# Attention, gated convolution and MLP on one core: Q, K and V laid out by kernel(), keys read in place for the first batch

## The reference

```
# attention: block 32, window 16
k_sum = k.reshape(B, H, nb, 32, D).max(axis=3)
v_sum = v.reshape(B, H, nb, 32, D).mean(axis=3)
local   = scale * q @ k.T          where |i - j| < 16, else -1e9
summary = scale * q @ k_sum.T + log(32)
a = softmax([local, summary]);   x = a @ [v, v_sum]
# gated convolution, x is (2, 768, 512), d_ff 1024
h = relu(x @ w_in);  g = sigmoid(conv3(h, conv_w));  x = (h * g) @ w_out
# MLP, 4 * 512 = 2048 hidden
out = x + relu(layernorm(x) * g_ln @ w_ch1) @ w_ch2
```

## Time and profile before

| what | before |
|---|---|
| median of three runs | 463.69 us |
| span of the profiled execution | 460.9 us |
| instructions | 8619 |
| DMA in all | 35.28 MB in 74725 packets, of which 57632 under 512 B |
| PE busy | 452.0 us |

### The profile page before, as it was taken

The page is one execution under the profiler, slowest core; times in us unless marked ns, Lnnn a source line. Parts: engine busy times, 40 slices in busy tenths (PEclk is TensorE's granted clock), DMA queues, the critical chain, the costliest instruction groups (busy, mean ns, idle before and its releaser), DMA issues.

```text
span 460.9 us, 8619 instructions
## 1 busy us (share of the span) xinstructions
PE 452.0 (98%) x3114; PEld 400.5 (87%) x3114; DVE 275.0 (60%) x630; ACT 200.1 (43%) x503; POOL 268.3 (58%) x405
## 2 busy tenths in 40 slices
PE   7899999999999999999999999999999999999997
PEld 6687888989989889989889988998998899889885
DVE  4999976876666967974674254546762244124333
ACT  3898997433335746436243143422421233123210
POOL 2559689999945000097898889750042687878000
PEclk9999999999999999999999999999999999999999
DMA  9998951212102000002115324120020211220003
GB/s 229 213 232 197 195 140 53 92 47 91 47 0 93 0 1 0 1 0 91 54 41 143 109 93 93 67 91 1 26 89 23 93 46 47 91 93 0 1 0 137
DMA packets 74725, 35.28 MB, mean 77 GB/s; under 512 B 57632, under 2 KB 68924, under 8 KB 74684
## 3 DMA queue, kind: packets, MB, share of 16 engines
q1 hardware_dynamic: 71164, 33.85, 27.1%
q10 hardware_dynamic: 3520, 0.88, 0.9%
HBM read 28.83 MB, written 3.15 MB: 69 GB/s over the span
## 4 chain that ended last, share of the span: by engine, by line
PE 96%; DMA 1%; DVE 1%; issue 1%; ACT 1%; ACTq 0%; DVEq 0%
PE two L1689 10%; PE two L1687 10%; PE two L1688 10%; PE two L1664 9%; PE two L1667 8%; PE two L1666 8%; PE two L1460 5%; PE two L1462 5%; PE two L1461 5%; PE two L1595 5%; PE two L1596 5%; PE two L1594 5%; PE two L1413 3%; PE two L1445 3%; PE two L1424 3%; PE two L1342 3%
## 5 line engine op out<-in xcount | busy, mean ns | idle before, releaser
L640 POOL TENSOR_TENSOR asum<-wst 128x256 f32<-128x256 f32 x26 | 21.8, 838 | 93.4 <-PE two L1462 50.2
L1664 PE MATMUL two<-combo,wa 128*128 128x384 f32 x224 | 75.8, 338 | 0.0
L1667 PE MATMUL two<-combo,wa 128*128 128x384 f32 x224 | 75.6, 337 | 0.0
L1666 PE MATMUL two<-combo,wa 128*128 128x384 f32 x224 | 75.2, 336 | 0.0
L1689 PE MATMUL two<-wv,h 128*128 128x512 f32 x192 | 75.0, 391 | 0.0
L1687 PE MATMUL two<-wv,h 128*128 128x512 f32 x192 | 74.8, 390 | 0.2 <-DVE h L946 0.2
L1688 PE MATMUL two<-wv,h 128*128 128x512 f32 x192 | 75.0, 390 | 0.0
L1023 DVE TENSOR_TENSOR u<-two,u 128x384 f32<-128x384 f32 x16 | 8.9, 558 | 90.2 <-PE two L1667 90.2
L1267 ACT ACTIVATE h<-u 128x384 fp32r<-128x384 f32 x16 | 8.4, 525 | 122.4 <-DVE u L1023 122.4
L574 POOL TENSOR_SCALAR pn<-ex,rinv 128x120 f32<-128x120 f32 x96 | 34.8, 383 | 19.1 <-DVE rinv L736 18.4
L634 POOL TENSOR_TENSOR wa<-asum,wa 128x256 fp32r<-128x256 f32 x52 | 43.2, 831 | 4.3
(11 more groups left out here) (119 smaller groups left out, 981.0 us busy)
## 6 DMA issues: line engine op xcount, KB each, us to landing
wst<-in_moe_w_ch SPq DMA_DIRECT2D x26, 512.0 KB, 3.2
vW<-in_v SPq DMA_DIRECT2D x13, 288.0 KB
kn<-in_k SPq DMA_DIRECT2D x15, 192.0 KB, 3.8
qn<-in_q SPq DMA_DIRECT2D x15, 192.0 KB, 3.7
out<-y SPq DMA_DIRECT2D x11, 256.0 KB, 2.0
wst<-in_moe_w_in SPq DMA_DIRECT2D x8, 256.0 KB, 3.1
wst<-in_moe_w_out SPq DMA_DIRECT2D x8, 256.0 KB, 2.8
tok<-xq SPq DMA_DIRECT2D x32, 48.0 KB, 2.0
```

Source lines behind the costliest of these rows:

```text
L1664: nc.tensor.matmul(o, wk[:, 0, kk], ck[:, 0, kk], start=(first and kk == 0), stop=False, skip_group_check=True)
L1666: nc.tensor.matmul(o, wk[:, 0, kk], ck[:, 1, kk], start=False, stop=False, skip_group_check=True)
L1667: ins = nc.tensor.matmul(o, wk[:, 1, kk], ck[:, 0, kk], start=False, stop=(kk == 1), skip_group_check=True)
```

## The change

kernel() now hands over other arrays: Q and K with two heads' 64 dimensions on 128 rows and tokens along the row (K with 16 zeros at each end), V as the 96-row windows of its 12 blocks packed in one row per partition (6 KB), conv_w and g_ln with 128 rows. So `keys_t`, `queries_t`, `queries`, `window_keys_0`, the transpose of the constants and their semaphores are gone, a DMA writes `kT`, `qT` and `vW` directly, one for each tensor of a pair, and there are four homes for K and three for Q. For pairs 0 to 3 `scores` reads 96 keys from `kT` and the 24 maxima from `ks` in two products with the same stationary block. For pairs 4 to 7 DVE copies the windows from `kT` to `kW` in one instruction, and POOL still adds the maxima. Scores of the first 12 groups use four PSUM banks in turn instead of two. `exps` waits for each block's maximum and no longer for all four. The orders of all five engines are written anew, up to chunk 5 of the gated convolution; `fill(i)` is three transposes of the identity, called 16 times. `warm(4)` is gone.

The diff, cut to its core:

```
 kernel():
+    def laid_out(name):
+        a = inputs[name]
+        if name in ("q", "k"):
+            a = a.transpose(0, 1, 3, 2).reshape(b * h // 2, 2 * d, s)
+        elif name == "v":
+            a = a.reshape(b, h // 2, 2, s, d).transpose(0, 1, 3, 2, 4).reshape(b * h // 2, s, 2 * d)
...
+        if name == "k":
+            a = _np.pad(a, ((0, 0), (0, 0), (win, win)))
+        elif name == "v":
+            a = _np.pad(a, ((0, 0), (win, win), (0, 0)))
+            rows = _np.arange(qb + 2 * win)[:, None] + qb * _np.arange(s // qb)
+            a = a[:, rows].reshape(len(a), qb + 2 * win, -1)
 scores_at():
-            return ps_s[j % 2][:, c:c + KW]
+            return bank[j % 2 + (6 if n < LATE and n % 2 else 0)][:, c:c + KW]
 SP:
+                sp.dma_start(kT[key_home(p)][:], k[p]).then_inc(k_in[key_home(p)], 16)
+                sp.dma_start(qT[p % 3][:], q[p]).then_inc(q_in[p % 3], 16)
+                sp.dma_start(vW[p % 3][0:KEYS].rearrange("p n d -> p (n d)"), v[p]).then_inc(v_in[p % 3], 16)
 DVE:
+            def window_keys(p):
+                dve.wait_ge(k_in[key_home(p)], key_in(p))
+                dve.wait_ge(s_ready, GPP * (p - 1))
+                nc.vector.tensor_copy(kW[p % 2][:, :, 0:KEYS], k_windows(p, 0, NQ)).then_inc(kw_done, 1)
 ACT, exps(n):
-                act.wait_ge(mx_done, GB * (n + 1))
                 for j in range(GB):
+                    act.wait_ge(mx_done, GB * n + j + 1)
 PE:
-            def transposes(src, dst, done):
-                for t in range(T):
-                    ins = nc.tensor.transpose(dst[:, TOK0 + P * t:TOK0 + P * (t + 1)],
-                                              src[:, t].rearrange("p h d -> p (h d)"), ident[:])
+            def fill(i):
+                c = P * (i % 4)
+                for k in range(3):
+                    nc.tensor.transpose(ps_o[2][:, c:c + P], ident[:], ident[:])
 scores(n):
-                    pe.wait_ge(mx_done, GB * n)
+                    pe.wait_ge(mx_done, GB * (n - 1 if n <= LATE else n))
+                        if p < PPB:
+                            nc.tensor.matmul(o[:, 0:KEYS], qb, kT[p][r, QB * b:QB * b + KEYS],
+                                             start=True, stop=True, skip_group_check=True)
+                            ins = nc.tensor.matmul(o[:, KEYS:KW], qb, ks[r, p % 2], start=True, stop=True, skip_group_check=True)
+                        else:
+                            ins = nc.tensor.matmul(o, qb, kW[p % 2][r, b], start=True, stop=True, skip_group_check=True)
 the written order of PE (...: calls left out), from probs_t(13) on:
+            probs_t(13)
+            hidden(0, [0, 1, 2, 3])
+            scores(17)
+            probs_t(14)
+            hidden(0, [4, 5])
...
+            probs_t(23)
+            project(0, [0])
+            project(0, [1])
+            project(0, [2])
+            outputs(22)
+            outputs(23)
+            hidden(4, [0, 1, 2, 3])
```

More of the change, by code:

```diff
@@ new lines, in _ @@
+            probs_t(1)
+            fill(8)
+            fill(9)
+            fill(10)
+            fill(11)
+            probs_t(2)
+            outputs(0)
+            outputs(1)
+            scores(6)
+            probs_t(3)
+            scores(7)
+            scores(8)
+            probs_t(4)
+            fill(12)
+            fill(13)
+            fill(14)
+            fill(15)
+            outputs(2)
+            block_means(2)
+            probs_t(5)
+            outputs(3)
+            outputs(4)
@@ new lines, in _ @@
+            scores(9)
+            probs_t(6)
+            scores(10)
+            scores(11)
+            block_means(3)
+            outputs(5)
+            probs_t(7)
+            outputs(6)
+            probs_t(8)
+            scores(12)
+            outputs(7)
+            probs_t(9)
+            outputs(8)
+            scores(13)
+            block_means(4)
+            probs_t(10)
+            scores(14)
+            outputs(9)
+            outputs(10)
+            probs_t(11)
+            scores(15)
@@ new lines, in _ @@
+            scores(19)
+            probs_t(17)
+            hidden(1, [2, 3])
+            outputs(15)
+            outputs(16)
+            scores(20)
+            probs_t(18)
+            hidden(1, [4, 5, 6, 7])
+            scores(21)
+            block_means(7)
+            outputs(17)
+            scores(22)
+            probs_t(19)
+            hidden(2, [0, 1, 2])
+            scores(23)
+            hidden(2, [3, 4, 5])
+            outputs(18)
+            outputs(19)
+            probs_t(20)
@@ L1600, in tokens_t @@
+            project(3, [3])
+            project(3, [4])
+            project(3, [5])
             def tokens_t(slot, dst):
```

754 lines of the change are left out of this document (354 added, 400 removed).

## The result

The changed kernel took 466.64 us (median of nine runs, 463.86 to 468.8) where the kernel before took 463.69 (nine runs, 462.73 to 467.02). The ratio is 1.0061, 95% interval 1.0037 to 1.0086: slower by 0.6%, where 1.1% faster was forecast. The span of the profiled execution grew from 460.9 to 466.7 us; it is one of the two slowest of the nine.

The account below looks back on a forecast made before the run. PE, busy 98% of the span, was taken as the bound, with three other limits close from 10 to 50 us. 13.0 + 4.1 - 6.3 - 2.8 - 0.9 - 1.8 = 5.3 us saved gave 458.4 us, range 453.8 to 464.0.

Parts of the forecast that it names:

- the new idle time: PE waits in the changed kernel: 1.8 us added (0.5 to 4), provided the other engines keep up.
- The old 4.1 us: PE's winnable idle time before 80 us in the kernel before, all expected to go.
- ScalarE's chain (29.5 us) and PE's (39 us): Work up to the first hidden products: ScalarE through at 37 us, PE at 44.7, so PE later by some 7 us.
- The step on DMA: Loads of Q, K and V: fewer, longer pieces lower the DMA share of 1.01, worth nothing beyond the start.
- The scores' term: First 12 score groups, split into 96 and 24 columns: 0.80 us a group instead of 0.57, 2.8 us added (0 to 6.8).
- Broken overlap: Rival in the split scores: a quarter's two products run one behind the other, 1.7 us a group, 469.2 us; chance 0.07.
- The slow start's 0.9 us: First scores start at 5.7 us and run at the slow clock until about 7.5 us: 0.9 us added (0 to 1.6).
- the slow clock lasts: Rival on PE from 7.5 to about 17 us: fillers do not hold the higher clock, some 6 us more, 464.4 us; chance 0.06.
- Transposes gone: PE loses 16 calls of six K or Q transposes and `warm(4)`: 13.0 us saved.
- fillers added: PE gains 16 calls of three identity transposes, 48 in all, at their full cost: 6.3 us added.
- ScalarE and POOL: Rivals: ScalarE bounds the second half, 462.0 us, chance 0.15; POOL's weight splits stall PE, 460.4 us, chance 0.10.
- The first hidden product: Sign in the changed kernel's profile, at the end of the attention's first half: expected at about 45 to 47 us.

Follow-up runs that it names:

- run 2: Changed kernel with two order swaps near 61 us: block keys of pair 6 before weight split 4, V of pair 6 loaded before the second weight; 464.57 us, 1.0037.
- run 4: Changed kernel with 21 of the 24 block-key products in groups 9 to 11 left out, 42 instructions fewer; 463.19 us, 0.9988 of the kernel before.
- run 6: Changed kernel with its large transfers spread by SP's order alone, and the maxima of key pair 3 later on DVE; 463.66 us, 1.0014.
- run 1: Changed kernel with the block means of pair 1 moved behind the transposes of group 1; 467.28 us, 1.0061 of the kernel before.
- run 7: Changed kernel with the edits of run 1, run 2 and run 6 together; 463.07 us, 0.9982 of the kernel before.
- run 15: The unedited changed kernel measured a second time; median 468.22 us of eight executions, beside 463.33 for the kernel before.
- run 16: Run 7's version with two SP waits at the start, pair 0's reload moved, V of pair 2 before pair 3's K and Q, K of pair 4 later; 460.22 us, 0.9941.
- run 9: Changed kernel with Q, K and V laid out so transfers go in pieces of 256, 320 and 512 bytes, same bytes and order; 465.34 us, 1.0032.
- run 11: Run 7's version with the transfers of Q, K and V in pieces of 256 to 512 bytes; 463.47 us, 1.0010 of the kernel before.
- run 5: Changed kernel without fillers 2 to 15 (42 transposes); 463.84 us, 1.0008 of the kernel before.
- run 8: Run 7's version without fillers 2 to 15; 462.47 us, 0.9981 of the kernel before.
- run 17: Run 16's version without fillers 8 to 15; 461.36 us, 0.9975 of the kernel before.
- run 3: Changed kernel with SP waiting for each large transfer to land before the next, V of pair 2 to Q of pair 5; 469.74 us, 1.0125.

## Why the prediction was wrong

**The step that failed is the new idle time, "1.8 us (0.5 to 4)", and with it the clock, which the sum had no term for after the start.** The old 4.1 us of idle time went and 10.4 us came, not 1.8. Against the spans the forecast was -5.3 us and the result +5.8, an error of 11.1 (8.2 by the medians, 458.4 forecast and 466.64 measured). By the pages, idle time should have changed by -4.1 + 1.8 = -2.3 us and changed by 15.2 - 8.9 = +6.3: 8.6 us. Busy time should have changed by -13.0 + 6.3 + 2.8 + 0.9 = -3.0 and changed by -0.5: 2.5 us.

*Why the idle time was mis-sized.* The working took ScalarE's chain (29.5 us) and PE's (39 us), found PE later by 7 us and concluded that others would keep up. They did: no wait of PE on ScalarE, VectorE or POOL is above 1.5 us, and the longest of them, 1.46 us, is at the start. What was not costed are the transfers. The step on DMA saw the share fall and ended at "worth nothing beyond the start"; it asked whether PE waits for a DMA today, not what long packets issued back to back do to another transfer, nor whether each load still comes before a PE that asks sooner. The share fell indeed, from 1.01 to 0.69, and the bytes up to 50 us from 10.8 to 9.7 MB (rates times lengths of the stretches); it is no matter of volume. The 3.3 us at 32.6 wait for a transfer that no line of the kernel issues. The 1.2 us on `kW` are order (run 2), and so is the part of the 1.9 us on V that falls at 62 us (run 2); the part at 14 us stood also in runs 4 and 6, and runs 1 and 7 show that behind it lay a late fetch.

*The scores' term, 2.8 us (0 to 6.8), came out at its lower end.* Starts in the changed kernel, `scores(2)` and `scores(3)`:

```profile
10.15 0.42 PE L1402 MATMUL two<-kT,qT 64*64 64x96 f32 x8
...
10.74 0.42 PE L1402 MATMUL two<-kT,qT 64*64 64x96 f32 x8
```

0.59 us a group, against 0.57 before and not 0.80: 0.2 us over 12 groups. The Trainium skill, TensorEngine Tiling (Array Packing), Instruction Overhead, would charge the 24 columns as 60 and give 0.74 us; by these rows it does not hold for products in four quarters that follow each other. Broken overlap did not happen. The price of the second product is elsewhere: 32 more instructions a group, which drain the fetched ones twice as fast (run 4).

*The slow start's 0.9 us did not come in this profile, and that is luck of one execution.* The change:

```profile
4.41 0.85 PE L1361 MATMUL two<-ident 128*128 128x128 f32 x6
6.72 0.42 PE L1402 MATMUL two<-kT,qT 64*64 64x96 f32 x8 [1.46 <-DVE ks L710]
```

The same kernel in run 15:

```profile
4.42 1.49 PE L1361 MATMUL two<-ident 128*128 128x128 f32 x6
5.90 0.62 PE L1402 MATMUL two<-kT,qT 64*64 64x96 f32 x8
```

In the change the six fillers take 0.85 us, 0.14 us each and not 0.218. PE then waits, since scores can start only at 6.72 and not at 5.7 us, and these run at the full clock. In run 15 the six take 1.48 us, and two groups of scores take from 5.90 to 8.01 us, 2.1 us where 1.2 would do: the 0.9 us of the forecast. Fifteen of the eighteen later profiles have the fillers at 1.48 or 1.49 us, three at 0.98 to 1.26. So the term was sound, and the time at which the clock rises differs between executions of one kernel. The Trainium skill, TensorE: Matmul & The Clock Gate, Part 4, holds that transposes do not bring the full clock; again the trace does not agree, since PE had run nothing else.

*The clock.* Run 16 has the same 3253 records, no low clock after the start, and 4.4 us less busy time (447.1 against 451.5). Its own start holds some 0.9 us of slow work that the change's profile was spared (1.5 us against 0.85 for the fillers, 1.6 against 1.3 for the scores behind them), so the low clock behind waits cost the change nearer 5.3 us (an estimate). The rival "the slow clock lasts" had the right engine and the wrong time: it did not last from the start; it came back at waits. In the kernel before it did not, and there the longest wait of PE after 5 us was 0.5 us. So busy time was off by +5.3 for the clock, -2.6 for the scores, -0.9 and -0.45 for the slow start and its six fillers, 1.35 in all; of the 2.5 us some 1.2 remain. Two groups differ up to 125 us. The transposes of the probabilities take more, before and then in run 16:

```profile
L1424 PE MATMUL two<-ident,pn 128*120 128x128 f32 x96 | 15.2, 281 | 0.1
```

```profile
L1418 PE MATMUL two<-ident,pn 128*120 128x128 f32 x96 | 17.4, 290 | 1.6 <-ACT pts L1078 1.1 <-POOL pn L571 0.3
```

The outputs take less, 16.2 us before and 14.5 in run 16 (15.4 in the change). A reading that fits the first is that PE now reaches the transposes before POOL is through with the four parts, and waits between them in pieces too small to count as idle. No run tries it, and the remainder stays open.

*Transposes gone, fillers added, ScalarE, POOL.* The terms of 13.0 and 6.3 us stand, as far as the busy time tells (18 fillers take 2.1 us, 0.117 us each). ScalarE and POOL bounded nothing, and the waits on ScalarE's copies in the second half are 0.7 us. The first hidden product was forecast for 45 to 47 us and came at 53.2; in run 16 it came at 47.6.

*Was the change sound?* With its transfers in another order, two waits of SP at the start and a few calls moved on PE, VectorE and POOL (run 16), it is 0.6% faster than the kernel before, where 1.1% was forecast. Its count of PE's work was right in the main, and its schedule, written for PE's waits, was late for the DMA queues.

**What stays open.** How much of the loss each cause has: the fetch, the orders and the low clock follow each other, and no run takes away the late fetch and leaves all else as it was. By how much packet length and by how much bytes ahead delay a fetch (runs 9 and 11 do not agree); which arbitration does it; and what of the scatter that is left (458.0 to 463.1 us in run 16) is fetches. Run 16 changed several orders at once, and I did not take its parts apart.

## What to carry to other kernels

When a change makes the bounding engine faster, list which transfers it will now want in the same few microseconds, by bytes and packets, beside the engines that must keep up; a DMA share that falls on average can still hide a backlog. A stall with no releaser in the middle of one call, once every 256 or so instructions, was here an instruction fetch: look which large transfers were issued just ahead of it, and move those that are not urgent into a quiet stretch, since taking the stall away by pacing only moved it to whoever stood behind the paced queue. And a wait of 1 to 3 us can cost more than its length, because the clock may fall with it; two edits that each remove one wait need not add.

## What the hardware showed unexpectedly

- A fetch of PE's instructions (16 KB, 0.9 to 2.3 us in transfer) began up to 4.9 us after the count at which it otherwise begins, when 1.5 MB of large packets were moving, and PE, where it had run dry, resumed 1.2 to 1.7 us after one had landed.
- The unedited change took 459.5 to 470.0 us over 21 executions; with the transfers in order, 458.0 to 463.1.
- Two products of 96 and 24 columns with the same stationary block, in four quarters of the array, cost a group the time of one of 120 (0.59 and 0.57 us), whereas 64 instructions instead of 32 were fetched.
- The granted clock fell to half in or up to 2 us behind waits of 0.9 to 5.5 us, for 3.4 or 6.8 us in most cases, and for 10.2 us in runs 5 and 8. It stayed full through other waits of that size: 1.1 us in run 16, 1.3 in run 11, 1.6 in run 17 (at 18.7 us) and 2.4 in run 3 (at 64.3 us).
- The time at which the clock first rises differs between executions of one kernel: in the change's profile the six fillers at 4.4 us took 0.85 us, in its other two profiles 1.49 us, and in run 15 the scores ran slowly up to 7.5 us.
